# Attention and two feed-forward layers on one core: the sums and low parts of x spread over more groups, and values loaded ahead of q and k

## The chip, the cores and the metric

The kernel runs on one core of a Trainium2 chip, in one launch. The time is the device time of one execution in microseconds (us). A run is compared by the median of several executions; beside them there is one profiled execution with a trace, from which all rows below come.

## The reference

```python
q_rot, k_rot = (rotate(q), rotate(k))                  # rope; batch 4, heads 8, 576 positions, head_dim 64
scores = scale * np.matmul(q_rot, k_rot.transpose(0, 1, 3, 2))
attn = softmax(scores)                                 # exp(scores - max), over sum + 1e-9
x = (attn @ v) as [2304 tokens, 512]
h = x @ w_in ;  g = h - np.tanh(h)  ;  x = g @ w_out   # first layer, w_in 512x2048, w_out 2048x512
h = x @ w_in2;  g = h * sigmoid(h)  ;  out = g @ w_out2
```

All is float32. The kernel keeps nearly the full precision by splitting each operand of a matmul into a rounded high part (type fp32r) and a low part (the operand less its high part), and by three matmuls for each product: low by high, high by low, high by high.

## The kernel before, in words

**Attention** runs over 16 pairs of heads (PAIRS), n = 0 to 15. For a pair, GpSimd (POOL) multiplies and adds the rope (`rope_scale`, `rope_add`: two multiplies, one for q and k with the cosines, one for the swapped copies with the sines, and an add) three pairs ahead. ScalarE (ACT) copies high parts of q and k (`qk_high`) and of v (`v_high`), POOL subtracts to get the low parts (`qk_low`, `v_low`). TensorE (PE) computes scores, ACT the exponentials, VectorE (DVE) the low part of the exponentials (`low`, tile pl) and the row maxima, PE the product with v. Then the sums are gathered by DMA, inverted, stored and spread to all partitions, and POOL's `normalise` writes x, transposed, into xT. All DMAs are issued by SyncE (SP), in one written order; a wait there holds back every DMA behind it. In the loop over n that order is: load q and k of pair n+3 (tile raw, one DMA of 1152 KB with four parts: q, k, swapped q, swapped k), load the split v of pair n+1 (tile vr), gather the sums of pair n-1 (waits until ACT has moved the second half of that pair out, s_ev), load the full v of pair n+1, join the two heads, store the maxima, store the inverse sums, copy blocks of the q and k of pair n+2, spread the inverse, and, for some n, load a part of the feed-forward weights (W_LOAD). vr has one buffer: v_high reads it in the midst of pair n, and ACT has the next exponentials queued behind that.

**The feed-forward part** has 6 tiles of 768 tokens (3 for each layer, `tile_of(g) = g // 8`) and for each tile 8 groups of 256 hidden units, 48 groups in all. A group's up product is done with one level of Strassen's scheme: 7 products (`product(g, i)`, i = 0 to 6) of sums of weight blocks with sums of x blocks, each with 6 matmuls (2 halves of k, 3 parts), into two PSUM banks in turn. ACT copies the result of product 0 out (`copy_first`), DVE adds the results of the others to sums (`add_product`, line 1195; 1 to 6, of which product 4 takes two adds). Product i+2 waits for the adds of product i, since it writes the same bank. Between the products PE runs the down products of the group before (`down_first`, `down_second`). ACT computes tanh, DVE the gate, ACT its high part, DVE its low part (`gate_low`, tile g_l). POOL makes the sums and low parts of the weights of the next group.

The x operands are made once for a tile: 7 high parts (`x_high(t, i)`, ACT, line 960) and 7 low parts (`x_low(t, i)`, DVE, line 1147; for tile 0 POOL makes numbers 0 to 3, line 528). Numbers 0, 1 and 6 are blocks of xT; 2 to 5 are sums of blocks, made by DVE's `x_sum(t, k)` (line 1143) in three buffers: k = 0 gives the source of number 4, k = 1 of number 2, k = 2 of number 3; k = 3 writes over buffer 0 and gives the source of number 5. The x of tile t+1 is made while tile t ends: in group 8t+6 the sums k = 0, 1, 2, one after the other, and in group 8t+7 all the rest. The first group of a tile can start product i only with x_l[i] there. There are five such turns, before groups 8, 16, 24, 32 and 40.

The order on each engine is that of the code. Semaphores: s_xh counts high parts of x, s_xl DVE's low parts, s_xp POOL's four, s_xt the sums, s_sm the adds, s_up the products.

## Time and profile before

| what | us |
|---|---|
| median of 3 runs | 1101.27 |
| lowest and highest | 1098.56, 1105.45 |
| the profiled execution, its own time | 1097.01 |
| its span in the trace | 1095.2 |

TensorE was busy for 1030.9 us of the span and had a mean granted clock of 0.979 of full speed. The attention part ends and the feed-forward part begins at 284 to 287 us. Times in the trace are us from the start of the span. The profiled execution was faster than the three timed runs by 1.5 to 8.4 us.

### The profile page before, as it was taken

The numbers are of one execution on the slowest core, as the hardware profiler recorded it, in microseconds if no ns is written. First come the engines' busy times: TensorE is split into PE (matmuls) and PEld (weight loads), VectorE is DVE, ScalarE is ACT, GpSimd is POOL, SyncE is SP. The second block draws the span as 40 slices with busy tenths as digits, with TensorE's granted clock in tenths as the row PEclk, the third lists the DMA queues.
The fourth block names the chain that finished last, engine by engine and source line by source line (L and its number), as shares of the span: only waits on it lengthen the run. The fifth ranks groups of instructions, "written<-read, shape, count | busy, mean of one in ns | idle before, by whom it ended". The sixth has DMA issues, their size and how long they took to land.

```text
span 1095.2 us, 17857 instructions
## 1 busy us (share of the span) xinstructions
PE 1030.9 (94%) x7116; PEld 934.4 (85%) x7116; DVE 639.3 (58%) x887; ACT 526.5 (48%) x791; POOL 719.7 (66%) x495
## 2 busy tenths in 40 slices
PE   3999999989799998999989999999989999899998
PEld 2889899889699988999889988888878888788887
DVE  6567676656544586445764467554675455844444
ACT  2567777767434434334353344543354442544432
POOL 6798999974576574765656766566756657466550
PEclk9999999989999998999999999899999999999999
DMA  5444554442111212212122212122121421113201
GB/s 180 156 135 158 191 177 148 153 140 63 53 61 56 78 39 77 77 42 74 45 72 77 71 46 77 39 78 77 39 78 40 135 77 62 54 40 134 78 20 57
DMA packets 66450, 94.56 MB, mean 86 GB/s; under 512 B 17088, under 2 KB 43968, under 8 KB 64448
## 3 DMA queue, kind: packets, MB, share of 16 engines
q1 hardware_dynamic: 66368, 93.43, 26.5%
q8 instruction: 56, 0.92, 0.3%
q14 instruction: 26, 0.21, 0.1%
HBM read 84.02 MB, written 4.79 MB: 81 GB/s over the span
## 4 chain that ended last, share of the span: by engine, by line
PE 71%; DVE 8%; DMA 6%; issue 5%; POOL 4%; SPq 3%; ACT 2%; DVEq 0%; ACTq 0%; POOLq 0%
PE ps L828 29%; PE ps L867 17%; PE ps L848 15%; DMA vr<-vin 4%; PE ps L693 3%; PE ps L657 2%; DVE xsum L1143 2%; PE ps L687 2%; DVE x_l L1147 2%; DMA raw<-qk 1%; DVE hid L1195 1%; POOL raw L479 1%; POOL raw L480 1%; PE ps L595 1%; SPq L377 1%
## 5 line engine op out<-in xcount | busy, mean ns | idle before, releaser
L524 POOL TENSOR_TENSOR win_l<-win_s,win_h 128x512 fp32r<-128x512 f32 x96 | 121.1, 1279 | 271.9 <-ACT win_h L951 271.9
L828 PE MATMUL ps<-x_h,win_l 128*128 128x384 f32 x672 | 230.6, 343 | 31.0 <-DVE hid L1195 13.8
L1011 ACT ACTIVATE th<-hid 128x768 f32<-128x768 f32 x96 | 80.5, 838 | 351.4 <-DVE hid L1195 351.4
L828 PE MATMUL ps<-x_l,win_h 128*128 128x384 f32 x672 | 229.5, 341 | 0.0
L828 PE MATMUL ps<-x_h,win_h 128*128 128x384 f32 x672 | 228.4, 340 | 0.0
L1195 DVE TENSOR_TENSOR hid<-ps,snap 128x384 f32<-128x384 f32 x192 | 106.4, 554 | 142.5 <-PE ps L828 142.5
L828 PEld LDWEIGHTS ps<-x_h,win_l 128*128 128x128 f32 x672 | 128.6, 191 | 48.8 <-DVE hid L1195 15.8
L1195 DVE TENSOR_TENSOR snap<-ps,snap 128x384 f32<-128x384 f32 x144 | 79.5, 552 | 123.0 <-PE ps L828 122.5
L1079 DVE TENSOR_REDUCE hm<-ps 128x2 f32<-128x576 f32 x144 | 108.4, 756 | 61.4 <-PE ps L595 53.4
L828 PEld LDWEIGHTS ps<-x_l,win_h 128*128 128x128 f32 x672 | 128.4, 191 | 10.3
L848 PE MATMUL ps<-g_l,wout_h 128*128 128x512 f32 (+1 forms) x384 | 131.8, 343 | 0.0
L848 PE MATMUL ps<-g_h,wout_h 128*128 128x512 f32 (+1 forms) x384 | 131.7, 343 | 0.0
L848 PE MATMUL ps<-g_h,wout_l 128*128 128x512 f32 (+1 forms) x384 | 130.7, 340 | 0.1
L524 POOL TENSOR_TENSOR wout_l<-wout_s,wout_h 128x1024 fp32r<-128x1024 f32 (+1 forms) x49 | 122.4, 2498 | 8.9 <-ACT wout_h L951 8.9
L828 PEld LDWEIGHTS ps<-x_h,win_h 128*128 128x128 f32 x672 | 128.2, 191 | 0.0
L524 POOL TENSOR_TENSOR win_l<-wsum,win_h 128x1024 fp32r<-128x1024 f32 (+1 forms) x50 | 122.5, 2451 | 0.0
L867 PE MATMUL ps<-wout_h,g_h 128*128 128x512 f32 x288 | 115.7, 402 | 0.0
L867 PE MATMUL ps<-wout_h,g_l 128*128 128x512 f32 x288 | 115.5, 401 | 0.0
L867 PE MATMUL ps<-wout_l,g_h 128*128 128x512 f32 x288 | 114.2, 396 | 0.6 <-DVE g_l L1212 0.5
L1018 ACT ACTIVATE g_h<-hid 128x768 fp32r<-128x768 f32 x96 | 81.0, 844 | 66.9 <-DVE hid L1203 33.6
L657 PE MATMUL ps<-hl 64*128 64x288 f32 x768 | 88.0, 330 | 6.0 <-DVE pl L1090 5.4
L848 PEld LDWEIGHTS ps<-g_h,wout_h 128*128 128x128 f32 x384 | 73.7, 192 | 8.4
(100 smaller groups left out, 2138.0 us busy)
## 6 DMA issues: line engine op xcount, KB each, us to landing
win_s<-w_in SPq DMA_DIRECT2D x45, 512.0 KB, 4.8
wout_s<-w_out SPq DMA_DIRECT2D x45, 512.0 KB, 3.8
raw<-qk SPq DMA_DIRECT2D x15, 1152.0 KB, 6.5
v<-vfull SPq DMA_DIRECT2D x16, 384.0 KB, 4.3
R<-inverse_sums SPq DMA_DIRECT2D x32, 144.0 KB, 3.0
vr<-vin SPq DMA_DIRECT2D x16, 192.0 KB, 6.1
out<-ostage SPq DMA_DIRECT2D x2, 1536.0 KB, 8.6
ev<-ev SPq DMA_DIRECT2D x16, 144.0 KB, 2.3
```

What stands on the lines that cost most here:

```text
L524: nc.gpsimd.tensor_tensor(lo, src, hi.bitcast(F32), ALU.subtract).then_inc(s_wl, 1)
L657: mm(ps[:, bank + h, 0:HALF], t[a, w, k], t[a, x, c], start=(w == KL), stop=False)
L687: last = mm(ps[:, OB + h, 0:HALF], v1[n % 2][a, WHOLE.index(i), h, :], P[whole_ring(g)][a, h, :], start=False, stop=final)
L693: last = mm(ps[:, OB + h, 0:HALF], w[n % 2][a, t, h, :], x[p][a, h, :], start=(first and m == 0), stop=False)
L828: last = mm(ps[:, up_bank(g, i), 0:TH], a[w][:, BLOCKS[i], kk, :], b[i][:, kk, :], start=(k == 0), stop=(k == 5))
L848: last = mm(flat[:, ACC + TN * d + lo:ACC + TN * d + up], x[w][:, f, 128 * d:128 * d + 128], y[:, f, lo:up], start=(j == 0 and f == 1 and ...
L867: last = mm(ps[:, 2 + c, :], y[:, f, 128 * c:128 * c + 128], x[w][:, f, :], start=(j == 0 and f == 1 and n == 0), stop=(j == NJ - 1 and f ...
L1011: nc.scalar.activation(th[:, f, :], hid[g % 2][:, f, :], ACT.Tanh, scale=(1.0, 0.5)[g // (NT * NJ)]).then_inc(s_t, 1)
L1018: nc.scalar.activation(g_h[:, f, :], hid[g % 2][:, f, :], ACT.Copy, scale=(1.0, 0.5)[g // (NT * NJ)]).then_inc(s_gh, 1)
L1079: nc.vector.tensor_reduce(o, ps[:, banks:banks + 2, 0:HALF], mybir.AxisListType.X, ALU.max, negate=True).then_inc(s_mx, 1)
L1143: nc.vector.tensor_tensor(o[:, :, :], a, b, ALU.subtract).then_inc(s_xt, 1)
L1195: nc.vector.tensor_tensor(to, ps[:, up_bank(g, i), 0:TH], other, ALU.add).then_inc(s_sm, 1)
```

## The change

1. In the feed-forward part, at the turn from tile t to t+1: the sums k = 0, 1, 2 stand one each in groups 8t+4, 8t+5 and 8t+6 (before the add of product 2) instead of all three in group 8t+6. Of the low parts, numbers 0 to 4 stay in group 8t+7, mostly a place or two later, and numbers 6 and 5, in this order, go to group 8t+8, the first of the new tile, with the sum k = 3. ACT's high parts 5 and 6 go there too. All seven low parts of tiles 1 to 5 are DVE's as before.
2. At the end of attention POOL makes x_l[0] in pair 14 and x_l[1] in pair 15, each before a `normalise`, instead of all four after the `normalise(14)` of pair 15.
3. On SP: the split v is loaded ahead of q and k; q and k are loaded by two DMAs with a semaphore each, of which the second (the swapped parts) is issued after `gather_sums`; the weights are loaded after the full v and ahead of `join_heads` instead of at the end of the iteration. `rope_scale` waits for the swapped half only ahead of its second multiply.

The core of the diff:

```diff
+        def x_highs(t, i):
+            return 7 * t + ((0, 1, 2, 3, 4, 5, 6) if t == 0 else (0, 1, 2, 3, 4, 6, 5)).index(i) + 1
+        X_POOL, X_DVE = (), (0, 1, 2, 3, 4, 6, 5)
+        def x_lows(t, i):
+            if t == 0:
+                return ("pool", i + 1) if i < 4 else ("dve", i - 3)
...
             def load(n):
                 sp.wait_ge(s_lq, n - 1)
-                sp.dma_start(raw[n % 2][:, :, :], qk[n, :, :, :]).then_inc(s_ld[n % 2], 16)
+                sp.dma_start(raw[n % 2][:, 0:2, :], qk[n, :, 0:2, :]).then_inc(s_ld[n % 2], 16)
+            def load_swapped(n):
+                sp.wait_ge(s_lq, n - 1)
+                sp.dma_start(raw[n % 2][:, 2:4, :], qk[n, :, 2:4, :]).then_inc(s_ls[n % 2], 16)
...
             for n in range(PAIRS):
+                if n + 1 < PAIRS:
+                    load_split_v(n + 1)
                 if n + 3 < PAIRS:
                     load(n + 3)
-                if n + 1 < PAIRS:
-                    load_split_v(n + 1)
                 if n >= 1:
                     gather_sums(n - 1)
+                if n + 3 < PAIRS:
+                    load_swapped(n + 3)
                 if 1 <= n < PAIRS - 1:
                     load_full_v(n + 1)
+                if n in W_LOAD:
+                    load_weights(*W_LOAD[n])
...
-                if n in W_LOAD:
-                    load_weights(*W_LOAD[n])
...
+                if n >= PAIRS - 2:
+                    x_low(n - PAIRS + 2)
                 if n >= 1:
                     normalise(n - 1)
-                if n == PAIRS - 1:
-                    for i in range(4):
-                        x_low(i)
+            x_low(2)
+            x_low(3)
             normalise(PAIRS - 1)
...                                              (DVE, the loop over groups; turn = j == 0 and g)
                 if g:
                     gate(g - 1, 0)
-                if ahead:
-                    x_low(t + 1, 0)
                 add_product(g, 1, first, h[:, 0, 0:TH], 0)
                 if g:
                     gate_low(g - 1, 0)
+                if NJ - 4 <= j < NJ - 1 and t + 1 < 2 * NT:
+                    x_sum(t + 1, j - NJ + 4)
+                if ahead:
+                    x_low(t + 1, 0)
+                if turn:
+                    x_sum(t, 3)
+                add_product(g, 2, first, u2, 0)
                 if ahead:
                     x_low(t + 1, 1)
-                if j == NJ - 2 and g + 2 < GROUPS:
-                    for k in range(3):
-                        x_sum(t + 1, k)
-                add_product(g, 2, first, u2, 0)
-                if ahead:
-                    x_low(t + 1, 2)
+                if turn:
+                    x_low(t, 6)
                 add_product(g, 3, u2, u3, 2)
-                if ahead:
-                    x_low(t + 1, 3)
+                if turn:
+                    x_low(t, 5)
                 add_product(g, 4, u3, h[:, 1, TH:TN], 3)
                 add_product(g, 4, u2, u4, 2)
                 if ahead:
-                    x_low(t + 1, 4)
-                    x_sum(t + 1, 3)
+                    x_low(t + 1, 2)
+                if ahead:
+                    x_low(t + 1, 3)
                 add_product(g, 5, u3, h[:, 1, 0:TH], 3)
-                if ahead:
-                    x_low(t + 1, 5)
                 gate(g, 1)
                 add_product(g, 6, u4, h[:, 0, TH:TN], 5)
                 gate_low(g, 1)
                 if ahead:
-                    x_low(t + 1, 6)
+                    x_low(t + 1, 4)
```

SP in iteration n = 6 of attention, before: raw is q and k of pair 9, vr the split v of pair 7, sums and ev the gathering and joining of pair 5, v the full v of pair 7, wout_s the weights.

```order
79 L361 DMA raw_91<-qk 128x2304
80 L366 DMA vr<-vin 128x384
81 L394 DMA sums<-ev_119 64x1x9 x2
82 L371 DMA v_113<-vfull 128x768
83 L398 DMA ev_119<-ev_119 64x576
84 L385 DMA mr_101<-rows 2x4x128
85 L386 DMA mr_101<-rows 2x1x64
86 L402 DMA inverse_sums<-rinv 128x9
87 L377 DMA hl_98<-hl_98 64x4x64 x2
88 L410 DMA R<-inverse_sums 64x576 x2
89 L357 DMA wout_s_53<-w_out 128x512
```

The same iteration of SP, changed:

```order
87 L385 DMA vr<-vin 128x384
88 L376 DMA raw_91<-qk 128x1152
89 L413 DMA sums<-ev_119 64x1x9 x2
90 L380 DMA raw_91<-qk 128x1152
91 L390 DMA v_113<-vfull 128x768
92 L372 DMA wout_s_53<-w_out 128x512
93 L417 DMA ev_119<-ev_119 64x576
94 L404 DMA mr_101<-rows 2x4x128
95 L405 DMA mr_101<-rows 2x1x64
```

vr now leads, the swapped half of raw stands behind the gathering of sums, and the weights stand ahead of the joining (ev) and the maxima (mr).

POOL at the end of attention (pairs 14 and 15), before: xT is `normalise`, x_l_62, 64, 66 and 68 are the low parts 0 to 3 of x.

```order
119 L496 TENSOR_TENSOR vl_117<-vr,vh_115 128x3x2x64
120 L524 TENSOR_TENSOR win_l_57<-wsum,win_h_56 128x512
121 L524 TENSOR_TENSOR win_l_57<-win_s_51,win_h_56 128x256
122 L502 TENSOR_TENSOR xT<-ev_119,R 128x576
123 L502 TENSOR_TENSOR xT<-ev_118,R 128x576
124 L528 TENSOR_TENSOR x_l_62<-xT,x_h_61 128x768
125 L528 TENSOR_TENSOR x_l_64<-xT,x_h_63 128x768
126 L528 TENSOR_TENSOR x_l_66<-xsum_74,x_h_65 128x768
127 L528 TENSOR_TENSOR x_l_68<-xsum_75,x_h_67 128x768
128 L502 TENSOR_TENSOR xT<-ev_119,R 128x576
```

POOL there, changed:

```order
121 L548 TENSOR_TENSOR win_l_57<-win_s_51,win_h_56 128x256
122 L552 TENSOR_TENSOR x_l_62<-xT,x_h_61 128x768
123 L526 TENSOR_TENSOR xT<-ev_119,R 128x576
124 L552 TENSOR_TENSOR x_l_64<-xT,x_h_63 128x768
125 L526 TENSOR_TENSOR xT<-ev_118,R 128x576
126 L552 TENSOR_TENSOR x_l_66<-xsum_74,x_h_65 128x768
127 L552 TENSOR_TENSOR x_l_68<-xsum_75,x_h_67 128x768
128 L526 TENSOR_TENSOR xT<-ev_119,R 128x576
```

Two of the four low parts now stand ahead of the normalise(14) (row 125) that POOL has to wait for.

DVE at the first turn, from the end of group 7 into group 8, before: hid and snap from ps are `add_product`, hid from hid and th is `gate`, g_l is `gate_low`, x_l_70, 72 and 77 are the low parts 4, 5 and 6.

```order
327 L1147 TENSOR_TENSOR x_l_70<-xsum_73,x_h_69 128x768
328 L1143 TENSOR_TENSOR xsum_73<-xT,xsum_74 128x768
329 L1195 TENSOR_TENSOR hid_83<-ps,snap_80 128x384
330 L1147 TENSOR_TENSOR x_l_72<-xsum_73,x_h_71 128x768
331 L1201 TENSOR_TENSOR hid_83<-hid_83,th 128x768
332 L1195 TENSOR_TENSOR hid_83<-ps,snap_81 128x384
333 L1210 TENSOR_TENSOR g_l<-hid_83,g_h 128x768
334 L1147 TENSOR_TENSOR x_l_77<-xT,x_h_76 128x768
335 L1201 TENSOR_TENSOR hid_83<-hid_83,th 128x768
336 L1195 TENSOR_TENSOR hid_82<-ps,snap_78 128x384
337 L1210 TENSOR_TENSOR g_l<-hid_83,g_h 128x768
338 L1195 TENSOR_TENSOR snap_79<-ps,snap_78 128x384
```

DVE there, changed:

```order
327 L1218 TENSOR_TENSOR hid_83<-ps,snap_80 128x384
328 L1224 TENSOR_TENSOR hid_83<-hid_83,th 128x768
329 L1218 TENSOR_TENSOR hid_83<-ps,snap_81 128x384
330 L1233 TENSOR_TENSOR g_l<-hid_83,g_h 128x768
331 L1170 TENSOR_TENSOR x_l_70<-xsum_73,x_h_69 128x768
332 L1224 TENSOR_TENSOR hid_83<-hid_83,th 128x768
333 L1218 TENSOR_TENSOR hid_82<-ps,snap_78 128x384
334 L1233 TENSOR_TENSOR g_l<-hid_83,g_h 128x768
335 L1166 TENSOR_TENSOR xsum_73<-xT,xsum_74 128x768
336 L1218 TENSOR_TENSOR snap_79<-ps,snap_78 128x384
337 L1170 TENSOR_TENSOR x_l_77<-xT,x_h_76 128x768
338 L1218 TENSOR_TENSOR snap_80<-ps,snap_79 128x384
```

Between the adds of products 5 and 6 (rows 327 and 329) only the gate is left, and the sum k = 3 and the low parts 6 and 5 stand among the adds of group 8.

## Rows read from the trace of the kernel before

**Rows 1.** Who TensorE waited for: us in total, times, longest wait

```profile
PE ps L828 <- DVE hid L1195: 13.8, 6, 2.6
PE ps L828 <- DVE snap L1195: 10.6, 5, 2.1
PE ps L657 <- DVE pl L1090: 5.4, 6, 2.8
PE ps L828 <- POOL x_l L528: 4.3, 2, 3.2
```

**Rows 2.** Timeline of ACT, copy_first of groups 2, 5 to 9 and 47: start, duration

```profile
316.07 0.49 ACT L1007 ACTIVATE snap<-ps 128x384 f32<-128x384 f32 x1 [1.19 <-PE ps L828]
...
363.31 0.49 ACT L1007 ACTIVATE snap<-ps 128x384 f32<-128x384 f32 x1 [1.19 <-PE ps L828]
...
379.05 0.49 ACT L1007 ACTIVATE snap<-ps 128x384 f32<-128x384 f32 x1 [1.20 <-PE ps L828]
...
397.17 0.49 ACT L1007 ACTIVATE snap<-ps 128x384 f32<-128x384 f32 x1 [1.19 <-PE ps L828]
...
417.87 0.47 ACT L1007 ACTIVATE snap<-ps 128x384 f32<-128x384 f32 x1
...
434.85 0.48 ACT L1007 ACTIVATE snap<-ps 128x384 f32<-128x384 f32 x1
...
1068.22 0.49 ACT L1007 ACTIVATE snap<-ps 128x384 f32<-128x384 f32 x1 [0.86 <-PE ps L828]
```

**Rows 3.** Timeline of DVE in group 5, an undisturbed one

```profile
367.49 0.56 DVE L1195 TENSOR_TENSOR snap<-ps,snap 128x384 f32<-128x384 f32 x1 [1.72 <-PE ps L828]
...
373.81 0.56 DVE L1195 TENSOR_TENSOR hid<-ps,snap 128x384 f32<-128x384 f32 x1 [1.09 <-PE ps L828]
...
376.16 0.55 DVE L1195 TENSOR_TENSOR hid<-ps,snap 128x384 f32<-128x384 f32 x1
377.16 0.96 DVE L1210 TENSOR_TENSOR g_l<-hid,g_h 128x768 fp32r<-128x768 f32 x1 [0.45 <-ACT g_h L1018]
```

**Rows 4.** The chain that ended last, at the first turn: start, us, what

```profile
377.97 2.10 PE ps L828 x12
...
416.15 2.29 PE ps L828 x6
418.44 3.73 PE ps L848 x12
```

**Rows 5.** Timeline of DVE in groups 6 and 7

```profile
381.43 2.05 DVE L1143 TENSOR_TENSOR xsum<-xT 128x768 f32<-128x768 f32 x1
...
384.82 3.12 DVE L1143 TENSOR_TENSOR xsum<-xT 128x768 f32<-128x768 f32 x1
...
415.54 0.55 DVE L1195 TENSOR_TENSOR hid<-ps,snap 128x384 f32<-128x384 f32 x1
```

**Rows 6.** Timeline of POOL in group 6, and of a like instruction in group 8

```profile
384.05 3.08 POOL L524 TENSOR_TENSOR win_l<-wsum,win_h 128x1024 fp32r<-128x1024 f32 x1
...
422.90 2.39 POOL L524 TENSOR_TENSOR win_l<-wsum,win_h 128x1024 fp32r<-128x1024 f32 x1
```

**Rows 7.** Timeline of POOL at the end of attention

```profile
284.30 5.00 POOL L528 TENSOR_TENSOR x_l<-xT,x_h 128x768 fp32r<-128x768 f32 x2
289.26 3.61 POOL L528 TENSOR_TENSOR x_l<-xsum,x_h 128x768 fp32r<-128x768 f32 x2
```

**Rows 8.** Timeline of ACT, and of TensorE, in pair 12's scores

```profile
229.13 0.52 ACT L905 ACTIVATE vh<-vr 128x384 fp32r<-128x384 f32 x1 [3.58 <-DMA vr<-vin]
...
231.58 1.08 PE L657 MATMUL ps<-hl 64*128 64x288 f32 x6 [2.82 <-DVE pl L1090]
```

**Rows 9.** Busy time by stretch, with PE's granted clock ahead of the DMA columns

```profile
225.00:240.00 15.00, 12.18 (x124) 10.76 (x122) 6.51 (x12) 6.50 (x14) 13.06 (x8) 0.77 0.42 141
```

**Rows 10.** DMA of the split v (16 of them): us from issue to landing

```profile
DMA to landing us min/median/max: 2.9/6.1/7.7
```

**Rows 11.** What SP waited for, at the gathering of sums

```profile
SPq L394 <- ACT ev L937: 36.1, 14, 5.0
```

More of the change, by code:

```diff
@@ L135, in attention_and_two_ffn @@
         s_ld = [sem(f"qk_loaded{i}") for i in range(2)]
+        s_ls = [sem(f"swapped_qk_loaded{i}") for i in range(2)]
         s_vr = sem("split_v_loaded")
@@ L323, in x_source @@
             return x_block(t, *kind[1:]) if kind[0] == "x" else xsum[kind[1]][:, :, :]
+        def x_highs(t, i):
[4 more added lines that the diff above has]
+                return ("pool", i + 1) if i < 4 else ("dve", i - 3)
+            if i in X_POOL:
+                return "pool", 4 + len(X_POOL) * (t - 1) + X_POOL.index(i) + 1
+            return "dve", 3 + len(X_DVE) * (t - 1) + X_DVE.index(i) + 1
         flat = ps[:, :, :].rearrange("p b c -> p (b c)")
@@ L418, in _ @@
             sp.dma_start(idf[:, :], ident).then_inc(s_id, 16)
-            sp.dma_start(raw[1][:, :, :], qk[1, :, :, :]).then_inc(s_ld[1], 16)
+            sp.dma_start(raw[1][:, 0:2, :], qk[1, :, 0:2, :]).then_inc(s_ld[1], 16)
+            sp.dma_start(raw[1][:, 2:4, :], qk[1, :, 2:4, :]).then_inc(s_ls[1], 16)
             load_split_v(0)
@@ L428, in _ @@
             load(2)
+            load_swapped(2)
             sp.wait_ge(s_lq, 2)
@@ L479, in rope_scale @@
                 nc.gpsimd.tensor_tensor(t[:, 0:2, :], t[:, 0:2, :], ctab[:, :, :].to_broadcast([128, 2, S]), ALU.mult).then_inc(s_step, 1)
+                pool.wait_ge(s_ls[n % 2], 16 * (n // 2 + (n % 2)))
                 nc.gpsimd.tensor_tensor(t[:, 2:4, :], t[:, 2:4, :], stab[:, :, :].to_broadcast([128, 2, S]), ALU.mult).then_inc(s_step, 1)
@@ L524, in weight_low, with x_low @@
                 nc.gpsimd.tensor_tensor(lo, src, hi.bitcast(F32), ALU.subtract).then_inc(s_wl, 1)
-            def x_low(i):
-                pool.wait_ge(s_xh, i + 1)
-                nc.gpsimd.tensor_tensor(x_l[i][:, :, :], x_source(0, i), x_h[i][:, :, :].bitcast(F32),
+            def x_low(i, t=0):
+                pool.wait_ge(s_xh, x_highs(t, i))
+                nc.gpsimd.tensor_tensor(x_l[i][:, :, :], x_source(t, i), x_h[i][:, :, :].bitcast(F32),
                                         ALU.subtract).then_inc(s_xp, 1)
@@ L820, in product @@
                 if g % NJ == 0:
-                    if t == 0 and i < 4:
-                        pe.wait_ge(s_xp, i + 1)
-                    else:
-                        pe.wait_ge(s_xl, 7 * t + i - 3)
+                    who, count = x_lows(t, i)
+                    pe.wait_ge(s_xp if who == "pool" else s_xl, count)
                 k = 0
@@ L1034, in _ @@
                 t, j = tile_of(g), g % NJ
-                ahead = j == NJ - 1 and g + 1 < GROUPS
+                ahead, turn = j == NJ - 1 and g + 1 < GROUPS, j == 0 and g
                 copy_first(g)
@@ L1040, in _ @@
                     gate_high(g - 1, 0)
+                if turn:
+                    x_high(t, 6)
                 if ahead:
@@ L1049, in _ @@
                     weight_high(g + 1, "S")
+                if turn:
+                    x_high(t, 5)
                 if ahead:
@@ L1139, in x_sum @@
                 if k == 3:
-                    dve.wait_ge(s_xl, 7 * t + 1)
+                    dve.wait_ge(s_xl, x_lows(t, 4)[1])
                 o, a, b = ((xsum[0], b12, b11), (xsum[1], b22, xsum[0][:, :, :]), (xsum[2], b22, b12),
@@ L1145, in x_low @@
             def x_low(t, i):
-                dve.wait_ge(s_xh, 7 * t + i + 1)
+                dve.wait_ge(s_xh, x_highs(t, i))
                 nc.vector.tensor_tensor(x_l[i][:, :, :], x_source(t, i), x_h[i][:, :, :].bitcast(F32),
@@ L1228, in _ @@
                 t, j = tile_of(g), g % NJ
-                ahead = j == NJ - 1 and g + 1 < GROUPS
+                ahead, turn = j == NJ - 1 and g + 1 < GROUPS, j == 0 and g
                 h = hid[g % 2]
@@ L1237, in _ @@
                     gate_low(g - 1, 0)
+                if NJ - 4 <= j < NJ - 1 and t + 1 < 2 * NT:
[5 more added lines that the diff above has]
+                add_product(g, 2, first, u2, 0)
                 if ahead:
                     x_low(t + 1, 1)
-                if j == NJ - 2 and g + 2 < GROUPS:
-                    for k in range(3):
-                        x_sum(t + 1, k)
-                add_product(g, 2, first, u2, 0)
-                if ahead:
-                    x_low(t + 1, 2)
+                if turn:
+                    x_low(t, 6)
                 add_product(g, 3, u2, u3, 2)
-                if ahead:
-                    x_low(t + 1, 3)
+                if turn:
+                    x_low(t, 5)
                 add_product(g, 4, u3, h[:, 1, TH:TN], 3)
@@ L1251, in _ @@
                 if ahead:
-                    x_low(t + 1, 4)
-                    x_sum(t + 1, 3)
+                    x_low(t + 1, 2)
+                if ahead:
+                    x_low(t + 1, 3)
                 add_product(g, 5, u3, h[:, 1, 0:TH], 3)
-                if ahead:
-                    x_low(t + 1, 5)
                 gate(g, 1)
```

2 lines of the change are left out of this document (removed).

## The prediction

> **What bounds the kernel now.** I read the engines' busy time first: TensorE is busy for 1030.9 of 1095.2 us, so whatever the change gains must come from the 64 us in which it is not, and from stretches with a low clock. The view of waits says who keeps it idle. Ahead of the up products it is DVE's adds: 13.8 + 10.6 us in eleven waits, the rest being POOL's first low parts of x (4.3) and DVE's low part of the exponentials (5.4) [rows 1]. The view counts idle time only. What a turn costs in all is read from the starts of copy_first, one for each group. An undisturbed group takes 379.05 - 363.31 = 15.74 us; at the first turn the steps are 18.12, 20.70 and 16.98 us [rows 2], so 2.4 us are lost by group 6, 5.0 by group 7 and 1.2 by group 8: 8.6 us. Over all, from group 2 to group 47, 45 steps take 752.15 us [rows 2] where 45 x 15.73 = 708 would do (in the second layer a step is 15.72), so the five turns cost **44 us**, 8.9 each.
>
> Why they do is seen on DVE. In group 6 the sums of x stand in a row ahead of the add of product 2; the last of them takes 3.12 us and the first 2.05 [rows 5]. Product 4 waits for that add. In group 7 DVE has seven low parts and a sum on top of its usual work, and the add of product 6 begins at 415.54 [rows 5], 18.4 us after copy_first(7), against 376.16 - 363.31 = 12.85 in group 5 [rows 2, 3]. Product 1 of group 8 waits for it and starts at 416.15. Then TensorE runs at its half clock for a while: 6 matmuls in 2.29 us and 12 in 3.73, where 12 take 2.10 at full clock [rows 4], which is 1.2 + 1.6 = 2.9 us of the 8.6.
>
> **Part 1, the sums of x.** A DVE instruction with two inputs in SBUF waits for POOL. The last sum was asked for at 384.82 while POOL's instruction ran from 384.05 to 387.13, and it ended at 387.94, which is 0.81 after POOL's end; the POOL instruction itself took 3.08 instead of 2.39 [rows 5, 6]. So each takes its turn, and one such DVE instruction costs at worst the rest of one POOL instruction and about 0.9 of its own. Now one sum for each of groups 4, 5 and 6 stands where the first stood: asked for 2.4 us after copy_first, it ended 4.4 after it [rows 2, 5]. The add of product 2 begins at 4.2 in an undisturbed group [rows 3]. Product 4 needs it only at about 7.3 (the add of product 5 begins at 10.5; that product started 1.05 earlier, and product 4 2.1 before that [rows 3, 4]). So three moved sums cost 0 each, covered by 2.6 us of slack, and the 2.4 us of group 6 go.
>
> **Part 2, the low parts, walked through.** Times are from copy_first(7). The low parts 0 and 1 have a slack of about 2.6 us each and cost nothing. The two adds of product 4 end at about 9.4. Then come low parts 2 and 3 in a row. Number 2 waits for POOL at worst 2.4 and takes 0.9: it ends by 12.7. Number 3 meets short POOL sums and ends between 13.1 and 14.1. The add of product 5 so begins 2.6 to 3.6 us late. Product 0 of group 8 needs it at 14.7 and still starts in time, barely. The add of product 6 begins 2.35 after that of product 5 [rows 3], at 15.5 to 16.5, and ends at 16.0 to 17.0, and product 1, due at 15.7, idles for **0.3 to 1.3 us**. gate_low begins 1.0 after the add of product 6 and takes 0.96 [rows 3]; the down product behind product 1 needs it, which is 0.4 more. In group 8 the low part 5 must be there for product 5 at about 26; the walk brings it there 0.1 us early to 0.3 late. The sum k = 3 and the low part 6 have a slack of 1 us or more. That leaves 0.7 to 2.0 us a turn; I take 1.3, and 0.3 for an occasional low clock, so 1.6 where 8.9 were: 5 x 7.3 = **36 us**.
>
> A rule of the Trainium skill speaks against the change here: "SBUF — State Buffer", section "SBUF: two separate sides", says that the port shared by VectorE and GpSimd is an exclusive lock held for a whole instruction. The rows agree on the lock (3.12 against about 0.9). It does not say who gets the port next; what would come of POOL getting it twice in a row is the second rival.
>
> **Part 3, the start of the feed-forward part.** POOL's low parts 0 and 1 took 5.00 us from 284.30, right behind the normalise it had waited for, and 2 and 3 took 3.61 to 292.87 [rows 7]. Number 0 and 1 now stand earlier, in time in which POOL waits for the inverse sums in pairs 14 and 15. Numbers 2 and 3 start at 284.3, beside the same DVE work, and end by 289.3. Product 3 can start 3.6 us earlier; the 3.2 us idle before product 0 [rows 1] goes, some of it coming back ahead of products 2 and 3. I take off 0.6 for a clock that may fall there: **3 us**.
>
> **Part 4, attention.** The split v takes 2.9 us from issue to landing when nothing is ahead of it and 6.1 in the median, behind q and k [rows 10]. As the first transfer it should land 3 to 4 us sooner, and no wait of ACT for v was longer than 3.58 [rows 8]. That one had the exponentials behind it, then DVE's low part, then 2.82 us of idle TensorE at 231.58 [rows 8], and a granted clock of 0.77 in 225 to 240 [rows 9]: about 2.8 us idle and 0.23 x 12.2 = 2.8 of clock. The other five waits for DVE's low part come to 5.4 - 2.8 = 2.6 [rows 1]. Bounds: 0 (something else is late next, or the long wait was an accident of this execution) and 8.2. The rows are nearer to the upper end, since the cause, v behind q and k, goes in every pair; I take **6 us**, as the long wait may be shorter in other executions. The page "DMA: Bandwidth & Descriptors", section "Queues, rings and completion order", of the Trainium skill says that descriptors are consumed in ring order; by that too vr gains by leading, and rows 10 agree.
>
> What pays for it: SP issues one DMA more in an iteration (about 0.5 us, SP has spare time). The swapped half of q and k now stands behind a wait of 36.1 / 14 = 2.6 us in the mean [rows 11], but POOL needs it only one multiply later than the first half, and the first half comes sooner. The maxima are stored behind the weights and the full v, which have had some 4 us by then. I cost these at nothing; the cover is POOL's lead of three pairs.
>
> **Sum.** 36 + 3 + 6 = 45 us, off the span of 1095.2 and the execution's own 1097.0. That execution lies 4 us below the median, by chance as far as I can see, so I take the sum off the median: 1101.3 - 45 = 1056.
>
> **Rivals.**
> *The clock falls behind the small idle times that are left* (15 in 100). The 2.1 us of idling in group 6 of the first turn [rows 1] brought none (the whole step is 2.4 us over), the 2.6 us and more ahead of product 1 did. If 1.3 to 1.7 us of idling in two pieces also bring 2.9 us of half clock at each turn [rows 4], a turn costs 4.6, the turns give 21 us, all 30: 1071.
> *POOL gets the port twice in a row* (5 in 100). Then low parts 2 and 3 take 3.1 us each [rows 5], the add of product 5 starts at 15.6, product 0 is late as well, product 5 of group 8 waits 2 us and the clock falls; a turn costs 8 us as now, and only 2 + 3 + 6 + 5 = 16 us are saved: 1085. Against it: in group 6 POOL gave way after each instruction.
> *Attention gains nothing* (15 in 100), since TensorE is nearly always busy there and POOL is for 13 of 15 us [rows 9], so that a wait for something else follows: 1062.
> *Slower* (3 in 100): the swapped half of q and k comes late. POOL is the next bound in attention. If that half, behind the wait for the gathering, made POOL idle in each of 13 pairs, the change loses from 39 / 13 = 3 us a pair on; at 5.0 us, the longest such wait [rows 11], it is 65 - 39 = 26 us slower: 1127. Against it is POOL's lead and that the wait is 2.6 in the mean.
>
> **How the numbers follow.** The forecast case, 1056, has 62 in 100 and itself spans 1047 (residue of a turn 0.7, all of attention) to 1066 (residue 2.0, attention 2). The range reaches to the first and third rival and stops short of the second: 1044 to 1074. A measurement of this kernel tells about 1% (11 us) from no change. Faster by more: 62 + 15 + 15 and nearly all of the second rival, 0.95; within 1%: 0.03; slower: 0.02, of the 3 for the slower rival.
>
> **What would show it.** Right: steps of copy_first of 15.7 us through groups 4 to 6 of each tile, a step of 17 or less behind group 7 and no step over 16.5 behind group 8; a last sum of 0.9 to 2.1 us; a granted clock near 1.0 in 408 to 424 us; the first up product of the feed-forward part within 1 us of attention's end; vr landing in about 3 us and no wait of ACT for it. Wrong: low parts of 3 us; waits of TensorE for a low part 5 (product 5 of a turn's first group); waits of POOL for raw at the second multiply; maxima rows late, with TensorE waiting at a pair's first scores.

## The result, and the profile after

The changed kernel takes 1047.29 us (median of 3, 1046.66 to 1047.57) against 1101.27 us before: ratio 0.951, 95% interval 0.947 to 0.955. The profiled execution has a span of 1045.8 us, 49.4 less than before, and a mean granted clock of 0.998 instead of 0.979. The three parts of the prediction can be told apart by two marks in each trace, the end of attention's last matmul and the starts of copy_first. Before: 283.78 us, copy_first(2) at 316.07, copy_first(47) at 1068.22. Now: 272.68, 303.98 and 1018.86. So attention gave 283.78 - 272.68 = 11.1 us, the start of the feed-forward part 32.29 - 31.30 = 1.0, the five turns 752.15 - 714.88 = 37.3, and what follows group 47 is the same (27 us).

The steps of copy_first at the first turn (ACT's timeline: start, duration), to be read beside [rows 2]:

```profile
366.96 0.49 ACT L1030 ACTIVATE snap<-ps 128x384 f32<-128x384 f32 x1 [0.65 <-PE ps L851]
382.71 0.49 ACT L1030 ACTIVATE snap<-ps 128x384 f32<-128x384 f32 x1 [0.66 <-PE ps L851]
400.50 0.47 ACT L1030 ACTIVATE snap<-ps 128x384 f32<-128x384 f32 x1
417.02 0.48 ACT L1030 ACTIVATE snap<-ps 128x384 f32<-128x384 f32 x1
431.68 0.49 ACT L1030 ACTIVATE snap<-ps 128x384 f32<-128x384 f32 x1 [0.58 <-PE ps L851]
...
1018.86 0.49 ACT L1030 ACTIVATE snap<-ps 128x384 f32<-128x384 f32 x1 [0.86 <-PE ps L851]
```

Group 6 now takes 15.75 us, as any other. Groups 7, 8 and 9 take 17.79, 16.52 and 14.66 (the copy out is late by ACT's queue and catches up): 1.75 us in all where there were 8.6. The second turn costs the same, the three later ones 1.1 to 1.2, the five together 7.0. DVE in groups 6 to 8 (timeline; [rows 3, 5] answer):

```profile
369.34 2.06 DVE L1166 TENSOR_TENSOR xsum<-xT 128x768 f32<-128x768 f32 x1
371.32 0.55 DVE L1218 TENSOR_TENSOR snap<-ps,snap 128x384 f32<-128x384 f32 x1
...
392.04 4.02 DVE L1170 TENSOR_TENSOR x_l<-xsum,x_h 128x768 fp32r<-128x768 f32 x2
395.98 0.55 DVE L1218 TENSOR_TENSOR hid<-ps,snap 128x384 f32<-128x384 f32 x1
...
398.90 0.54 DVE L1218 TENSOR_TENSOR hid<-ps,snap 128x384 f32<-128x384 f32 x1
...
407.69 1.03 DVE L1170 TENSOR_TENSOR x_l<-xsum,x_h 128x768 fp32r<-128x768 f32 x1
```

One sum takes 2.06 us and the add behind it (of product 2) begins 4.4 us after copy_first(6) (366.96), in time for product 4: the sum costs nothing. In group 7 the low parts 2 and 3 take 4.02 us together; the add of product 5 begins 13.3 us after copy_first(7), that of product 6 16.2 after it in the first two turns and 15.6 in the other three. Who TensorE waited for (us in total, times, longest), beside [rows 1]:

```profile
PE ps L851 <- DVE hid L1218: 4.5, 6, 1.1
PE ps L851 <- POOL x_l L552: 3.1, 2, 1.9
PE ps L718 <- ACT ev L960: 2.5, 2, 1.2
```

What SP's queue waited for at the gathering, beside [rows 11]:

```profile
SPq L413 <- ACT ev L960: 38.5, 15, 4.4
```

The wait for snap is no longer listed, and that for DVE's low part of the exponentials (pl) is down to one of 1.0 us. Landing of the split v, beside [rows 10], and busy time by stretch with the granted clock, beside [rows 9]:

```profile
DMA to landing us min/median/max: 2.7/3.4/6.7
```

```profile
225.00:240.00 15.00, 13.77 (x187) 13.18 (x186) 9.61 (x16) 11.28 (x20) 13.13 (x10) 1.00 0.29 79
...
408.00:424.00 16.00, 16.00 (x94) 14.93 (x93) 10.87 (x13) 7.71 (x10) 13.33 (x9) 1.00 0.21 67
```

POOL at the end of attention (beside [rows 7]), where the low parts 2 and 3 now begin right behind the normalise that waited 9.38 us:

```profile
272.63 1.44 POOL L526 TENSOR_TENSOR xT<-ev,R 128x576 f32<-128x576 f32 x1 [9.38 <-DMA R<-inverse_sums]
274.02 5.01 POOL L552 TENSOR_TENSOR x_l<-xsum,x_h 128x768 fp32r<-128x768 f32 x2
```

### The profile page after: what moved, and what is told of

It is laid out like the page before. It is cut to its first block, busy times and chain, and to the rows that moved or that the text cites. A ratio compares the mean times of both kernels' runs of the same rounds, so it can differ in the third digit from the quotient of the medians.

```text
span 1045.8 us, 17872 instructions
## 1 busy us (share of the span) xinstructions
PE 1009.0 (96%) x7116; PEld 921.0 (88%) x7116; DVE 649.1 (62%) x887; ACT 528.1 (51%) x791; POOL 731.5 (70%) x495
## 4 chain that ended last, share of the span: by engine, by line
PE 86%; DVE 6%; POOL 3%; ACT 2%; DMA 1%; issue 1%; SPq 0%; ACTq 0%; DVEq 0%; POOLq 0%
PE ps L851 31%; PE ps L871 18%; PE ps L890 18%; PE ps L718 5%; PE ps L682 4%; PE ps L712 3%; DVE x_l L1170 2%; PE ps L620 2%; PE ps L684 1%; PE ps L672 1%; DVE hm L1102 1%; PE ps L748 1%; ACT th L1034 1%; ACT g_h L1041 1%; PE ps L638 1%
## 5 line engine op out<-in xcount | busy, mean ns | idle before, releaser
L548 POOL TENSOR_TENSOR win_l<-win_s,win_h 128x512 fp32r<-128x512 f32 x96 | 131.5, 1388 | 222.6 <-ACT win_h L974 222.6
L851 PE MATMUL ps<-x_h,win_l 128*128 128x384 f32 x672 | 227.4, 338 | 7.7 <-DVE hid L1218 4.5
L851 PEld LDWEIGHTS ps<-x_l,win_h 128*128 128x128 f32 x672 | 126.7, 189 | 10.6
L548 POOL TENSOR_TENSOR wout_l<-wout_s,wout_h 128x1024 fp32r<-128x1024 f32 (+1 forms) x49 | 115.4, 2355 | 8.9 <-ACT wout_h L974 8.9
L548 POOL TENSOR_TENSOR win_l<-wsum,win_h 128x1024 fp32r<-128x1024 f32 (+1 forms) x50 | 119.3, 2386 | 0.0
```

What stands on the lines that cost most here:

```text
L548: nc.gpsimd.tensor_tensor(lo, src, hi.bitcast(F32), ALU.subtract).then_inc(s_wl, 1)
L851: last = mm(ps[:, up_bank(g, i), 0:TH], a[w][:, BLOCKS[i], kk, :], b[i][:, kk, :], start=(k == 0), stop=(k == 5))
```

## The experiments

The experiments ran in three batches, each with its own runs of the kernel before beside it. These had medians of 1098.61 us (beside turn_only, loads_only, pool_only and low3_behind_add5), 1100.50 (beside v_first_only, halves_only, weights_only and sums_only) and 1101.33 (beside the rest). So a kernel of one batch is compared with one of another by the ratio to before, not by the median. The marks of a row are from one trace each. Two numbers in the expectations of the first batch are off: I had taken 274.8 us for the end of attention in the changed kernel and hence 9 us for the gain, where the trace has 272.68 and 11.1. In each run four marks are read: the end of attention, the time from there to copy_first(2), the time from copy_first(2) to copy_first(47) less 45 undisturbed steps (707.9 us; below: the turns), and the step behind groups 6 and 7.

| kernel | ratio to before, 95% interval | median | attention ends | to copy_first(2) | turns |
|---|---|---|---|---|---|
| before (first trace) | 1 | 1101.27 | 283.78 | 32.29 | 44.3 |
| changed (first trace) | 0.951 (0.947 to 0.955) | 1047.29 | 272.68 | 31.30 | 7.0 |
| turn_only | 0.965 (0.962 to 0.969) | 1062.09 | 286.65 | 32.98 | 7.0 |
| loads_only | 0.991 (0.988 to 0.994) | 1090.06 | 274.14 | 33.54 | 46.5 |
| pool_only | 0.997 (0.995 to 1.000) | 1096.31 | 283.08 | 30.91 | 46.6 |
| low3_behind_add5 | 0.949 (0.946 to 0.952) | 1043.57 | 273.76 | 29.04 | 3.0 |
| v_first_only | 0.993 (0.991 to 0.995) | 1092.51 | 277.18 | 32.38 | 45.0 |
| halves_only | 0.990 (0.987 to 0.993) | 1089.30 | 273.41 | 32.59 | 42.5 |
| weights_only | 0.997 (0.995 to 0.999) | 1097.79 | 283.80 | 33.09 | 46.0 |
| sums_only | 0.982 (0.980 to 0.984) | 1080.05 | 285.63 | 32.03 | 25.9 |
| lows_only | 0.976 (0.972 to 0.979) | 1076.06 | 283.30 | 32.38 | 19.3 |
| changed_again | 0.949 (0.946 to 0.952) | 1045.77 | 274.51 | 28.83 | 5.9 |
| short_pool_holds | 0.946 (0.944 to 0.949) | 1043.16 | 273.46 | 31.77 | 0.6 |
| halves_and_turns | 0.949 (0.947 to 0.952) | 1046.09 | 274.16 | 29.28 | 5.9 |

### The three parts, each alone

**turn_only** is the kernel before with the DVE, ACT and semaphore edits of the turns, and nothing of SP's or of POOL's order (the diff of parts 1 and 2 above, whole).

> The kernel before with part 1 and 2 of the change alone: the sums of x over three groups and the low parts over two; loads and POOL's order at the end of attention as before. Theory (the parts are independent and each gives what the trace shows): the 45 steps from copy_first(2) to copy_first(47) fall from 752.2 to 715 us and nothing ahead of group 2 moves, so about 37 us less than before by the profiled executions: 1064 by the run's own time, ratio 0.966. Rival (the turns' excess is made in part by TensorE's clock, which other stalls bring down too): steps of 17.5 us and more stay behind groups 6 and 7, and the gain is 21 us or less, ratio 0.98.

Measured: ratio 0.965; the turns cost 7.0 us, the steps behind group 7 are 17.2 to 17.8. For the turns the theory holds to 0.3 us in the trace (714.9 us for the 45 steps); that nothing ahead of group 2 moves does not hold, as attention ended at 286.66 here, 2.9 us later than in the first trace of before, in code that is the same. The rival's bound on the time lies above the whole interval.

**loads_only** is the kernel before with all of SP's edits and the second wait of `rope_scale`.

> The kernel before with SP's part alone: split v first, q and k in two halves, weights ahead of the joining. Theory: all of the 9 us that the changed kernel gains up to the end of attention (TensorE's last matmul of attention at about 274.8 instead of 283.8), the rest as before: about 1088 us, ratio 0.991. Rival (the one long wait for v in pair 12 of the trace of before was an accident of that execution): about 4 us, ratio 0.996. Turns stay at 8.9 us each.

Measured: ratio 0.991; attention ends at 274.14, the turns are as before (46.5). The rival falls: the gain is not that of one accidental wait. It comes back in every trace: with the old order of loads attention ended at 283.8, 286.7, 283.1, 283.8, 285.6 and 283.3 us (mean 284.4; weights_only, the fourth, is counted here), with the new one or with the halves beside the turns at 272.7, 274.1, 273.8, 274.5, 273.5 and 274.2 (273.8). ACT's waits for v came to 11.8 us in the trace of before and to more in that of turn_only (ACT's waits in 20 to 290 us: us in total, times, longest):

```profile
ACT vh L917 <- DMA vr<-vin: 14.2, 10, 3.1
```

**pool_only**:

```diff
+                if n >= PAIRS - 2:
+                    x_low(n - PAIRS + 2)
                 if n >= 1:
                     normalise(n - 1)
-                if n == PAIRS - 1:
-                    for i in range(4):
-                        x_low(i)
+            x_low(2)
+            x_low(3)
```

> The kernel before with POOL's low parts 0 and 1 of x ahead of the last normalises, alone. Theory: group 2 starts 3 us earlier after the end of attention (29.2 us behind its last matmul instead of 32.3), nothing else moves: ratio 0.997. Rival (product 3 waits for something else, or a low clock takes the gain back): 0 to 1 us, ratio 1.000.

Measured: 30.91 us to copy_first(2), 1.4 less than in the first trace of before, ratio 0.997 with an interval that ends just under 1.000 (0.9997). One trace can't settle 3 us here: the eight traces with POOL's old order have 32.0 to 33.5 us (mean 32.7), the five with the new one and DVE's start unchanged 31.3, 30.9, 29.0, 28.8 and 29.3 (mean 29.9). So it is worth 2.8 us in the mean, and the spread is large. Only 1.1 us of it is idle time: from attention's end to copy_first(2) TensorE idles for 4.9 us in the mean of the eight and for 3.8 in that of the five. The rest goes with the clock: over that stretch the granted clock was 0.90 to 0.95 of full speed in all of the eight, 0.95 in two of the five and 1.00 in the other three. In the changed kernel's first trace it was 0.91 in 272 to 290 us, in that of changed_again 1.00 (busy time by stretch):

```profile
272.00:290.00 18.00, 13.75 (x63) 11.93 (x61) 11.79 (x14) 5.30 (x8) 11.94 (x8) 0.91 0.20 56
```

```profile
272.00:290.00 18.00, 14.63 (x78) 12.58 (x77) 13.27 (x17) 5.86 (x10) 10.58 (x6) 1.00 0.24 68
```

### What of the loads gains

**v_first_only**:

```diff
+                if n + 1 < PAIRS:
+                    load_split_v(n + 1)
                 if n + 3 < PAIRS:
                     load(n + 3)
-                if n + 1 < PAIRS:
-                    load_split_v(n + 1)
```

> The kernel before with one edit on SP: the split v is loaded ahead of q and k, which stay one transfer; weights at the iteration's end. Theory (ACT's waits for v and what follows them are the steady part of attention's gain): no wait of ACT for v over 0.5 us behind pair 1, pairs 7 to 15 at 14.7 us each; attention ends 7 to 8 us earlier than in the kernels with the old order of loads (283.1 to 286.7 us in three traces), about 277: ratio 0.993. Rival (the halves and the weights' place carry it): under 3 us, ratio 0.998 or more.

Measured: attention ends at 277.18, 7.2 us before the old order's mean; no wait of ACT for v but the first pair's. The time is as the theory has it, the pace only in part: of the steps from one copy of the maxima to the next, the five behind pair 6 take 14.7 to 15.0 us, but the two after them 15.1 and 15.5, where the changed kernel's seven all take 14.7.

**halves_only**:

```diff
-                sp.dma_start(raw[n % 2][:, :, :], qk[n, :, :, :]).then_inc(s_ld[n % 2], 16)
+                sp.dma_start(raw[n % 2][:, 0:2, :], qk[n, :, 0:2, :]).then_inc(s_ld[n % 2], 16)
+            def load_swapped(n):
+                sp.wait_ge(s_lq, n - 1)
+                sp.dma_start(raw[n % 2][:, 2:4, :], qk[n, :, 2:4, :]).then_inc(s_ls[n % 2], 16)
...
                     gather_sums(n - 1)
+                if n + 3 < PAIRS:
+                    load_swapped(n + 3)
```

The loads of pairs 1 and 2, which stand ahead of the loop, are cut in two in the same way, here and in the changed kernel.

> The kernel before with q and k loaded by two DMAs, the second behind the gathering of sums, v behind the first half, weights at the end. Theory: POOL starts the first pairs about 1 us earlier each (2.8 us by pair 3 in the changed kernel's trace against before), and v lands sooner, as only half of the bytes are ahead of it; together 5 to 7 us: ratio 0.995. Rival (halves give nothing, since POOL still waits for the second): 0 to 1 us, ratio 1.000.

Measured: 273.41, 11.0 us before the old order's mean, more than I expected and as much as all of SP's edits together. v lands in 4.8 us in the median here (6.1 before), and ACT waits four times for it, 0.48 us at most. The rest of the gain is at the head. POOL's first multiply waited 8.30 us for the load of pair 1 before, and 6.55 in the changed kernel's trace:

```profile
11.80 2.63 POOL L479 TENSOR_TENSOR raw<-raw,ctab 128x1152 f32<-128x1152 f32 x1 [8.30 <-DMA raw<-qk]
...
29.36 2.65 POOL L479 TENSOR_TENSOR raw<-raw,ctab 128x1152 f32<-128x1152 f32 x1 [3.54 <-DMA raw<-qk]
```

```profile
10.04 2.96 POOL L502 TENSOR_TENSOR raw<-raw,ctab 128x1152 f32<-128x1152 f32 x1 [6.55 <-DMA raw<-qk]
...
27.22 2.64 POOL L502 TENSOR_TENSOR raw<-raw,ctab 128x1152 f32<-128x1152 f32 x1 [2.83 <-DMA raw<-qk]
```

By the copy of the maxima of pair 5 the six traces with the old loads stand at 104.6 to 107.1 us (mean 106.0), the six with the new ones at 101.8 to 104.1 (103.3), and halves_only at 102.3. That is 2.8 us of the gain ahead of pair 5. v_first_only stands at 103.7 there, so that POOL's earlier first multiply is not its only cause; I did not separate them further. From there to attention's end halves_only takes 171.1 us, v_first_only 173.5, the six new ones 170.5 in the mean and the six old ones 178.3. So the halves give some 2.4 us more than v's earlier landing there too. What else they do is that SP waits 16.8 us in all for the gathered sums to land, ahead of `join_heads`, instead of 41.6 before and 47.8 in v_first_only; whether the 2.4 us come from that, no run shows.

**weights_only**:

```diff
                     load_full_v(n + 1)
+                if n in W_LOAD:
+                    load_weights(*W_LOAD[n])
                 if n >= 1:
                     join_heads(n - 1)
...
-                if n in W_LOAD:
-                    load_weights(*W_LOAD[n])
```

> The kernel before with the weights' load alone moved from the iteration's end to behind the full v. Theory: the loads of q, k and v are issued 0.6 us earlier in the twelve iterations that have one behind them, ACT's waits for v shrink by that: 2 to 3 us, ratio 0.998. Rival: nothing, or up to 2 us lost where maxima and joining now queue behind 256 KB: ratio 1.000 to 1.002.

Measured: attention ends at 283.80, and ACT waits for v as before (11.8 us in 10 waits). The median is 2.7 us lower, at the edge of what the interval tells (0.995 to 0.999), and the trace shows no place for it. I take it for not shown.

**halves_and_turns** is the changed kernel without v first and without the weights' new place.

> The changed kernel without two of its edits on SP: the split v stays behind the first half of q and k, and the weights' load stays at the iteration's end. Theory (the halves alone carry what attention gains, as the first half ahead of v is short enough): the same as the changed kernel within 1.5 us, attention ends at 272.5 to 274.5 us. Rival (v first matters beside the halves): 2 us or more above it, with waits of ACT for v in several pairs.

Measured beside changed_again: 1046.09 against 1045.77 us, attention ends at 274.16 against 274.51, one wait of ACT for v of 0.45. A second wait, the first pair's, is 0.48. The rival falls: with the halves, v's place and the weights' place are worth nothing that can be measured. Two edits each remove nearly all waits for v; the second to be made finds them gone.

### What of the turn gains

**sums_only**:

```diff
-                if j == NJ - 2 and g + 2 < GROUPS:
-                    for k in range(3):
-                        x_sum(t + 1, k)
+                if NJ - 4 <= j < NJ - 1 and t + 1 < 2 * NT:
+                    x_sum(t + 1, j - NJ + 4)
```

> The kernel before with the sums of x in three groups alone, the low parts all in group 8t+7 as before. Theory (the two stalls of a turn are separate): the step behind group 6 falls to 15.75 us, those behind groups 7 and 8 stay at 20.7 and about 17; the five turns cost 30 us instead of 44 to 47: ratio 0.986. Rival (the sums' lateness is what makes group 7 late): the step behind group 7 falls too, under 18, ratio 0.97. Second rival (the clock saved in group 6 falls later instead): only 5 us, ratio 0.995.

Measured: the step behind group 6 is 15.75 in all turns, the one behind group 7 stays at 20.72, as the theory says; but the turns cost 25.9 us, not 30. ACT's timeline at the first turn:

```profile
380.65 0.49 ACT L1007 ACTIVATE snap<-ps 128x384 f32<-128x384 f32 x1 [0.64 <-PE ps L828]
396.40 0.49 ACT L1007 ACTIVATE snap<-ps 128x384 f32<-128x384 f32 x1 [0.64 <-PE ps L828]
417.12 0.47 ACT L1007 ACTIVATE snap<-ps 128x384 f32<-128x384 f32 x1
431.99 0.48 ACT L1007 ACTIVATE snap<-ps 128x384 f32<-128x384 f32 x1
```

The 20.72 is the same as before, but the next step is 14.87 where it was 16.98 [rows 2], and the granted clock is 1.00 in both windows of 395 to 432 us (busy time by stretch, first two lines). So this turn costs 4.0 us, and of the 8.6 before, 2.4 were the sums' stall and 2.1 a low clock behind group 7 that is missing here. That it is missing is no effect of the edit that can be relied on: in the other four turns of sums_only the clock does fall behind group 7 (third line, the fourth turn, where the step is 17.22), and they cost 5.1 to 6.1 us; in the first turn of halves_only, with the sums' stall still there, it does not fall there, and the step is 14.88.

```profile
395.00:412.00 17.00, 16.57 (x95) 15.15 (x94) 15.43 (x15) 9.30 (x14) 12.31 (x7) 1.00 0.12 40
412.00:432.00 20.00, 17.32 (x98) 15.60 (x97) 12.53 (x17) 10.94 (x16) 11.48 (x10) 1.00 0.23 73
...
807.00:824.00 17.00, 16.37 (x68) 14.55 (x69) 8.64 (x14) 7.35 (x11) 9.79 (x8) 0.82 0.18 63
```

**lows_only** is turn_only with the three sums left together in group 8t+6 (the diff above, backwards).

> The kernel before with the low parts of x over groups 8t+7 and 8t+8 as in the change, but the three sums together in group 8t+6 as before. Theory (two separate stalls, of which the sums alone took away 20 us): the step behind group 6 stays at 18.1 or 19.7 us, the one behind group 7 falls from 20.7 to about 17.5, and the five turns cost 24 to 28 us instead of 44 to 47: ratio 0.982. Rival (with group 6 late, group 7 stays late or TensorE's clock stays low into it): over 19 us behind group 7, ratio 0.99 or more.

Measured: behind group 6 18.1 us (19.7 once), behind group 7 17.2, the turns cost 19.3 us, less than I expected. Against a mean of 45 us in the six traces with the old turns the sums alone save 19, the lows alone 26, both 38 to 39, so that some 6 us are counted in each of the two. The steps behind groups 6 to 9 say where they are, by an estimate worked out from them. With the old turns the 45 us are 12 of stall behind group 6 (five times 2.4), 4.6 of low clock there (the step is 19.6 to 19.7 instead of 18.1 in 18 of the 30 turns), and 28.4 behind groups 7 to 9, some 20 of them lateness (the 4.0 of the turn above, five times) and the rest low clock. In lows_only the low clock in group 6 came in one turn of five. The instructions up to there are the same as before, so those 3 us are chance and not the edit. The other 3 are the smaller loss behind groups 7 to 9 in sums_only, 25.7 instead of 28.4 us; one trace does not show whether that is the edit or chance.

### What is left of a turn

**low3_behind_add5**:

```diff
                 if ahead:
                     x_low(t + 1, 2)
-                if ahead:
-                    x_low(t + 1, 3)
                 add_product(g, 5, u3, h[:, 1, 0:TH], 3)
+                if ahead:
+                    x_low(t + 1, 3)
                 gate(g, 1)
```

> The changed kernel with x_low(t+1, 3) moved from ahead of the add of product 5 to behind it, into the 0.9 us in which DVE waits for tanh. Theory (what is left at a turn, 1.1 to 1.75 us, is the add of product 5 coming 2.8 us late behind two low parts that each wait for POOL): the add of product 5 starts 1 to 2 us earlier, the add of product 6 0.5 to 1 us earlier, and a turn loses 0.5 us less or more: 2 to 5 us below the changed kernel in all. Rival (a low part in the gap delays the gate by as much): the same time as the changed kernel within 1 us.

Measured: the add of product 5 begins at 393.39, 11.9 us after copy_first(7) instead of 13.3, and that of product 6 14.7 after it instead of 15.6 to 16.2; the turns cost 3.0 us instead of 5.9 to 7.0. The ratio to before is 0.949, the same as that of changed_again, so the 3 us are shown by the traces' steps, not by the times. The low part 2 alone, in front of that add, and POOL's instruction under way (DVE's and POOL's timelines):

```profile
390.86 2.60 DVE L1170 TENSOR_TENSOR x_l<-xsum,x_h 128x768 fp32r<-128x768 f32 x1
393.39 0.54 DVE L1218 TENSOR_TENSOR hid<-ps,snap 128x384 f32<-128x384 f32 x1
```

```profile
390.25 2.40 POOL L548 TENSOR_TENSOR wout_l<-wout_s,wout_h 128x1024 fp32r<-128x1024 f32 x1
```

**changed_again** is the changed kernel, unaltered, beside the same runs of before as the last two kernels.

> The changed kernel itself, unaltered, beside the next two: 1047 us, ratio 0.951; a turn costs 1.1 to 1.75 us, 7 in all.

Measured: 1045.77 us; each turn 1.1 to 1.25, 5.9 in all. **short_pool_holds** adds to low3_behind_add5:

```diff
+                if g >= 2 and name in ("S", "O"):
+                    m = 4 if name == "S" else 1
+                    nc.gpsimd.tensor_tensor(lo[:, 0:m], src[:, 0:m], hi[:, 0:m].bitcast(F32), ALU.subtract)
+                    nc.gpsimd.tensor_tensor(lo[:, m:2 * m], src[:, m:2 * m], hi[:, m:2 * m].bitcast(F32), ALU.subtract).then_inc(s_wl, 1)
...
             x_sum(0, 3)
+            dve.wait_ge(s_xp, 4)
             x_low(0, 5)
             x_low(0, 6)
```

> The changed kernel with three edits: low part 3 behind the add of product 5 (as run before); POOL's low parts of 1024 columns in two instructions of 512 each from group 2 on; at the start of the feed-forward part DVE's low parts 5 and 6 wait for POOL's four. Theory (a DVE instruction with two SBUF inputs waits for the rest of the POOL instruction under way, not for POOL as such): low part 2 of a turn takes 1.0 to 1.9 us instead of 2.6, a turn costs 0 to 0.4 us instead of 0.6; POOL's two low parts at the start take 3.6 us instead of 5.0 and group 2 starts 1 us earlier behind the end of attention. 3 to 5 us under the changed kernel in all, ratio about 0.947. Rival (POOL gets the port again between its own instructions): low part 2 still takes 2.6 us, and only the other two edits show, about 4 us under the changed kernel less 1 for POOL's longer work.

Measured: the low part 2 takes 1.64 us instead of 2.60, as POOL's instruction under way is now 1.30 long and not 2.40 (DVE's and POOL's timelines):

```profile
393.30 1.64 DVE L1175 TENSOR_TENSOR x_l<-xsum,x_h 128x768 fp32r<-128x768 f32 x1
394.86 0.54 DVE L1224 TENSOR_TENSOR hid<-ps,snap 128x384 f32<-128x384 f32 x1
```

```profile
392.82 1.30 POOL L550 TENSOR_TENSOR wout_l<-wout_s,wout_h 128x512 fp32r<-128x512 f32 x1
394.08 2.01 POOL L551 TENSOR_TENSOR wout_l<-wout_s,wout_h 128x512 fp32r<-128x512 f32 x1
```

DVE asked at 393.30, POOL's first ended at 394.12, DVE ended 0.82 later, and POOL's second took 0.7 longer than the first: each takes its turn. The rival falls. The five turns cost 0.6 us in all. The third edit cost time. POOL's low parts take 3.62 us instead of 5.0, as expected, but DVE's low parts 5 and 6 then stand in front of the add of product 1, and TensorE waits there:

```profile
280.36 0.45 PE L856 MATMUL ps<-x_h,win_l 128*128 128x384 f32 x1 [3.03 <-DVE hid L1224]
```

From attention's end to copy_first(2) it takes 31.8 us instead of 28.8. In all the kernel is 2.6 us below changed_again (1043.16 against 1045.77, beside the same runs of before; ratios 0.946 and 0.949, intervals that overlap), where I had expected 3 to 5. Without the third edit it should gain some 3 us more; that is an estimate from the 31.8 and 28.8, and was not run.

## Why the prediction was right

I forecast 1056 us in a range of 1044 to 1074; the median is 1047.3. The sum was 36 + 3 + 6 = 45 us; the traces show 37.3 + 1.0 + 11.1 = 49.4, and the median fell by 54.0. So the forecast was 9 us too high, about half by attention (5.1 us) and half by the median of before (4.6). The measured time stands at the lower end of what I called the forecast case (1047), and changed_again's 1045.8 below it: the width of the range covered two gains that I had sized too small.

*Part 1, the sums.* Right: one sum in a group costs 0, and the walk's 4.4 us for its end is what the trace has. What they are worth alone is 19 us in five turns and not five times the 2.4 that I gave the stall in the first turn: 12 are the stalls, 4.6 a low clock within group 6 that the first turn happened not to have, and 3 less loss behind group 7, which one trace shows.

*Part 2, the low parts.* The walk was right step by step: the add of product 5 at 13.1 to 14.1 us, measured 13.3; the add of product 6 at 15.5 to 16.5, measured 15.6 to 16.2; a residue of 0.7 to 2.0 a turn, measured 1.1 to 1.75; 36 us, measured 37.3 to 38.4 (the traces of the changed kernel, turn_only, changed_again and halves_and_turns have 5.9 to 7.0 us left). Two of the signs that I had named were set a little too low: I wanted a step of 17 us or less behind group 7 and none over 16.5 behind group 8, and they are 17.2 to 17.8 and 16.5. The step behind group 9 gives back 1.1 us, so the residue is still within the walk's. The low part 5 of the new tile was no stall (it ended at 408.7, 8.2 us after copy_first(8), where product 5 is due at 9.4 or later). The allowance of 0.3 for the clock was not needed: in groups 6 to 9 of all five turns the granted clock stayed at 1.00.

*Part 3, the start.* The size was right in the mean (2.8 us over several traces, 3 foretold; 1.0 in the changed kernel's first trace), but by luck in its make-up. I had 3.6 us of waiting gone and 0.6 taken off for the clock. The traces have only 1.1 us less idle time, since TensorE still waits for POOL's low parts (3.1 us in two waits, where it was 4.3), and the rest comes from a clock that was low in all eight traces with the old order and at full speed in three of five with the new one.

*Part 4, attention.* The direction was right, and so was the cause for most of it: v lands in 3.4 us instead of 6.1, ACT waits for it no more after the first pair, and v first alone gives 7.2 us. The size is the term that was off: 6 us, upper bound 8.2, measured 11.1, and 10.6 between the means of six traces each. Two things were missed. The halves were costed at nothing, with POOL's lead as cover; ahead of pair 5 there is no such lead yet, and 2.8 us are gained there. And from pair 5 on the gain is 7.8 where I took 6. In three traces with the old loads (pool_only, weights_only and lows_only) the granted clock was 1.00 from there on, and they lose 6.1 to 6.6 us against the mean of the new ones; in the other three it was 0.98 to 0.99 and they lose 8.4 to 11.0. So 6 us was about right for an execution without a low clock, and the low clock, which was 2.8 of my 8.2, comes on top in some executions only.

*The median.* I took the sum off the median of before, though its profiled execution lay 4 us lower. In other traces of kernels with the old turns the step behind group 6 is 19.6 to 19.7 us, with a low clock, in two to four turns of five, where the first trace had it in two. That and the waits for v may be what a median of before carries over its best execution; there is no trace of a slower execution of before, so it is not shown. The runs fit it: six runs of changed_again lie within 4.9 us, the eleven of before beside them within 11.5.

*The rivals.* The clock did not fall behind the small idle times left at the turns (1.1 us at most). I had put little on that, because the 2.1 us of idling in the first turn had brought no low clock; that reading rested on one turn, since the same stall has a step of 19.7 us in the second and fifth turn of the same trace. POOL did not get the port twice in a row; DVE did wait for a POOL instruction under way, as foretold, and short_pool_holds shows that it ends with the instruction under way. Attention gained more than nothing. The swapped half was not late: SP waits 38.5 / 15 = 2.6 us at the gathering, as before, and POOL shows no wait for it at the second multiply.

## What to carry to other kernels

A periodic surplus of work that stalls the bounding engine in one place can be free when it is cut into pieces each shorter than the slack of the step behind it; work the slack out from an undisturbed period and walk the new order through it. Price the low clock behind a stall as a chance, from several like places, and not from one: the same stall of 2.1 us was followed by it in 18 of 30 turns here, and each time it cost 1.5 us more. Where VectorE and GpSimd both work from SBUF, look at the longest GpSimd instruction that a VectorE instruction may meet: one low part of VectorE took 2.60 us beside a GpSimd instruction of 2.40 and 1.64 beside one of 1.30. A small transfer that someone needs soon (192 KB here) should not stand behind a large one (1152 KB) on the same queue. Moving the small one ahead gave 7.2 us and cutting the large one in two 11.0 (one trace each, ratios 0.993 and 0.990); with the second done, the first added nothing.

## What the hardware showed that I had not expected

The same stall is not followed by the same clock. Behind the 2.1 us of idling in group 6 the step was 18.1 us in 12 of the 30 turns with the old order and 19.6 to 19.7 in the other 18, where the granted clock over the step was 0.91. Behind the lateness of group 7, which is 20.7 us in all 30, the next two steps lose between nothing and 2.4 us more by the clock. Over five turns the low clock made up some 13 of the 45 us that the old turns cost, by the estimate under lows_only.
